# Twelve small ScalarE operations in place of two GpSimd operations, for three of the 24 units of a recurrent-attention and mixture kernel

## The chip, the cores and the metric

The kernel runs on one core of one Trainium2 chip. The metric is the device time of one execution in microseconds (us), the median of several runs. The text calls the engines TensorE (PE in the profile), VectorE (DVE), ScalarE (ACT), GpSimd (POOL) and SyncE (SP, which only issues DMAs here).

## The reference

Three stages follow each other; the inputs are fp32.

```python
batch, n_heads, seq, head_dim = (4, 8, 768, 48)
for t in range(S):
    cur = np.einsum('bhd,bhe->bhde', u[None] * kt, vt)
    y[:, :, t] = np.einsum('bhd,bhde->bhe', rt, state + cur)
    state = wt[:, :, :, None] * state + np.einsum('bhd,bhe->bhde', kt, vt)
# y as x of 3072 x 384
h = x @ w_in                              # 384 x 2048
x = (h * np.clip(h + 3.0, 0.0, 6.0) / 6.0) @ w_out
# soft mixture: 3072 tokens, 32 slots, 8 experts (384 -> 1024 -> 384)
logits = x @ phi
slot_input = softmax(logits over tokens).T @ x
slot_out[e] = np.maximum(slot_input[e] @ w1[e], 0.0) @ w2[e]
out = softmax(logits over slots) @ slot_out
```

Two terms of the first stage matter for the change. The part of `y` from `cur` is a diagonal term: for each token and head, the sum over `d` of `r*u*k`, times `v`. And the state is multiplied by the product of `w` over a chunk of tokens before the next chunk adds to it.

## The kernel before, in words

**Units.** The sequence is cut into six chunks of 128 tokens. A unit `n` is one chunk of one batch: `n = 4*chunk + batch`, 24 units (`UNITS`), counted from 0. `B` is 4 and `SPLIT` is 8. Units 0 to 3 (the first chunk) and most of unit 4 run ahead of the main loop. Units 5, 6 and 7 are the sixth to eighth.

**Steps.** The main loop runs over `s` = 0 to 100. The first 96 are steps of the first matrix product (`mlp(s)`: nine matmuls of 128x512 into `hid`). Every engine has its own copy of the loop and its own fixed order of work. Step `s` belongs to unit and phase `divmod(s + 19, 4)`, so four steps go by for a unit: step 0 is phase 3 of unit 4, steps 1 to 4 are phases 0 to 3 of unit 5, steps 5 to 8 of unit 6, steps 9 to 12 of unit 7, and from step 13 on come the units from 8. All engines run their queues in order, and semaphores with fixed counts tie them together.

**A unit's work.** VectorE scans the decays in both directions (`scan_suffix`, `scan_prefix`; from unit 8 on `open_prefix` with the scan at L962 and `close_suffix` with the scan at L975). GpSimd multiplies keys and receptance by the scans (`decay_keys` L1678, `decay_receptance` L1690). TensorE makes scores (`score`), VectorE masks them (`mask_scores` L1016), ScalarE rounds them to 16 bits (`high_scores` L1380) and GpSimd takes the rest (`low_scores` L1669). `v` is split likewise: `high_v` on ScalarE, `low_v` on VectorE (L1059) for units 4 to 7 and on GpSimd later. `attend` (matmuls from L575) needs the low scores, the low `v` and the decayed state. VectorE adds the diagonal term in `finish_y` (L1035), TensorE turns the result (`turn_x`, L599) and ScalarE and VectorE write it as input of `mlp`. In `increment` TensorE forms what VectorE adds to the state.

**The diagonal term.** GpSimd multiplies `r*k*u` in `diag_products` (L1634, L1636), VectorE sums each head (`sum_diag` L1055, into `diag`, 8 columns), and GpSimd multiplies `v` by it in `diag_values` (L1663, one operation of 128x384, into `diag_v`). `finish_y(n)` waits for it, and SyncE waits for `diag_v_done` before it loads a later unit's natural rows. For units 0 to 3 ScalarE does it with eight operations of 128x48 in `first_diag_values` (L1468), each of which takes one column of `diag` as its scale.

**The state.** For units 4 to 7 GpSimd decays it in `decay_state` (L1705, one operation of 112x384). From unit 8 on ScalarE does, with four operations of 112x96 (`decay_new_state`, L1409).

**The split of the weights.** In the first steps `w_in` is still being split into high and low halves in pieces: ScalarE makes the high one (`high_w`, L1445) and scales the piece (`scale_w`, L1451), behind its work of steps 0, 4, 5, 8 and 9; GpSimd makes the low one (`low_w`, L1648), at the end of its work of steps 1, 2, 5, 6, 9 and 10.

**Per step.** After `mlp(s)`, ScalarE takes `relu_step(s)` (L1473), VectorE `gate(s)` (L1075) and a transpose (L1096); `mlp(s)` needs `gate(s - 2)`. VectorE takes `gate(s)` behind its unit work of the same step.

Of the kernel before, what the change touches and what calls it, by code (L numbers as in the profile page):

```python
# [6 lines left out]
ACT = mybir.ActivationFunctionType  # L7
# [4 lines left out]
P = 128  # L12
# [13 lines left out]
B, H, S, D = 4, 8, 768, 48  # L26
# [3 lines left out]
PB = H // 2  # L30
# [3 lines left out]
PD = ALIGN + D  # L34
# [13 lines left out]
SPLIT = 2 * B  # L48


def build_program(nc, wT, rkT, nat_in_dram, u, u_blocks, w_in, w_outT, w_out, phi, w1, w2, out):
    with ExitStack() as ctx:
        def sb(name, cols, dt=F32):
            return ctx.enter_context(nc.sbuf_tensor(name, [P, cols], dt))

        def sem(name):
            return ctx.enter_context(nc.semaphore(name))
# [4 lines left out]
        def carve(n):  # L62
            at[0] += n
            assert at[0] <= 15872
            return att[:, at[0] - n:at[0]]

        def pairs(ap, n):
            return ap.rearrange("p (i n) -> p i n", n=n)
# [4 lines left out]
        suffix, prefix, restart, mark = (carve(SCAN) for _ in range(4))  # L73
# [11 lines left out]
        diag_v = carve(DM)  # L85
        y_nat = carve(DM)
        state = [pairs(carve(PB * 2 * D), 2 * D) for _ in range(B)]
# [20 lines left out]
        diag = sb("diag", H)  # L108
# [22 lines left out]
        def r_dec_of(n):  # L131
            return r_dec[n % 2 if n < SPLIT else 0]
# [7 lines left out]
        def nat_rows_of(n):  # L140
            return nat_early.get(n, nat[n % 2])
# [25 lines left out]
        def nat_of(n, which):  # L167
            return nat_rows_of(n)[:, which * DM:(which + 1) * DM]
# [89 lines left out]
        state_copied = sem("state_copied")  # L258
        suffix_done = sem("suffix_done")
# [4 lines left out]
        decayed = sem("decayed")  # L264
# [3 lines left out]
        v_scaled = sem("v_scaled")  # L268
# [11 lines left out]
        y_done = sem("y_done")  # L280
# [9 lines left out]
        diag_done = sem("diag_done")  # L290
        diag_v_done = sem("diag_v_done")
# [75 lines left out]
        def unit_of(s):  # L367
            return divmod(s + 4 * B + 3, 4)

        def is_unit(n):  # L370
            return 0 <= n < UNITS

        def scaled_behind(s):
            return {0: 3, 4: 4, 5: 5, 8: 6, 9: 7}.get(s)

        def split_behind(s):
            return {1: 2, 2: 3, 5: 4, 6: 5, 9: 6, 10: 7}.get(s)
# [987 lines left out]
        def _(act):  # L1365
# [23 lines left out]
            def copy_keys(n):  # L1389
                act.wait_ge(k_turned, n + 1)  # L1390
                if n:
                    act.wait_ge(inc_ready, 2 * n)
                scale = Y_SCALE * R_SCALE if n < B else Y_SCALE if n < SPLIT else Y_SCALE / V_SCALE
                nc.scalar.activation(k_nat, k_ps[:, 0:PB * PD], ACT.Copy, scale=scale).then_inc(k_nat_done, 1)
# [9 lines left out]
            def decay_new_state(n):  # L1404
# [4 lines left out]
                    last = nc.scalar.activation(s, s, ACT.Copy, scale=chunk_decay[n % B][0:PD, p:p + 1])  # L1409
                last.then_inc(decayed, 1)  # L1410

            def high_receptance(n):
                act.wait_ge(r_dec_done, n + 1)
                act.wait_ge(y_ready, n)
                nc.scalar.activation(r_hi[0:PD], r_dec_of(n)[0:PD], ACT.Copy).then_inc(r_hi_done, 1)

            def high_state(n):
                if n < SPLIT:
                    act.wait_ge(state_added, n - B + 1)
                else:  # L1420
                    act.wait_ge(decayed, n - B + 1)
                    act.wait_ge(y_ready, n + 1)
                nc.scalar.activation(state_hi[n % B][0:PD], state[n % B][0:PD], ACT.Copy).then_inc(state_hi_done, 1)
# [57 lines left out]
            def copy_logit_parts(g):  # L1481
                act.wait_ge(l_ready, 16 * g + 16)
                if g:
                    act.wait_ge(folded, g)
                if g < C - 1:
                    nc.scalar.activation(l_hi, l_ps[:], ACT.Copy).then_inc(l_hi_done, 1)
                else:
                    nc.scalar.activation(l_part[:, EARLIER], last_l[0], ACT.Copy).then_inc(l_part_done, 1)
                    act.wait_ge(late_l_ready, 4)
                    nc.scalar.activation(l_part[:, LATER], last_l[1], ACT.Copy).then_inc(late_l_part_done, 1)  # L1490
# [57 lines left out]
            for s in range(END):  # L1548
                n, phase = unit_of(s)
                g, i = divmod(s, FT)  # L1550
                if phase == 0:
                    if g >= 1 and i == 1:
                        copy_logit_parts(g - 1)
                    if is_unit(n):
                        high_v(n)
                        if n >= SPLIT:
                            high_receptance(n)
                if phase == 1:
                    if is_unit(n - 1):
                        high_x(n - 1)  # L1560
                    if 1 <= g < C and i == 2:
                        weigh(g - 1)
                    if is_unit(n):
                        high_scores(n)
                if phase == 2:
                    if n < LAST_INC:
                        copy_keys(n)
                    if SPLIT <= n + 1 < UNITS:
                        save_decay(n + 1)
                    if SPLIT - B <= n - 2 < LAST_INC:  # L1570
                        high_state(n - 2)
                if phase == 3 and SPLIT <= n - 1 < LAST_INC:
                    decay_new_state(n - 1)
                if s < STEPS - 1:
                    relu_step(s)
                elif s == STEPS - 1:
                    for half in range(2):
                        last_relu(half)
                if s == 0:
                    copy_keys(B)  # L1580
                c = scaled_behind(s)
                if c is not None:
                    high_w(c)
                    scale_w(c)
                if g == C and i == 2:
                    weigh(C - 1)
                    copy_logits(C - 1)
                if s == STEPS - 10:
                    c_exp(0)
                if s == STEPS - 5:  # L1590
                    c_high(0)
# [7 lines left out]
            for q in range(KT):  # L1599
                cols = slice(q * P, (q + 1) * P)  # L1600
# [14 lines left out]
            for half in range(2):  # L1615
                act.wait_ge(stack_ready, half + 1)
                nc.scalar.activation(stack[0:3 * SLOTS, MODEL[half]], bank[4 + half][0:3 * SLOTS, 0:DM // 2], ACT.Copy,
                                     scale=SLOT_SCALE).then_inc(stack_hi_done, 1)
            for i in range(1, UNITS, 2):
                act.wait_ge(final_ready, i + 1)  # L1620
                if i // 2 >= OUT_PAIRS:
                    act.wait_ge(stored[i // 2 % OUT_PAIRS], 32 if i // 2 % OUT_PAIRS < SINGLE else 16)
                nc.scalar.activation(out_pair[:, i // 2 % OUT_PAIRS, 1, :], bank[4 + i % 4][:, 0:DM], ACT.Copy,
                                     scale=1.0 / (SLOT_SCALE * SOFT_SCALE)).then_inc(final_done[1], 1)

        @block.gpsimd
        def _(pool):
# [73 lines left out]
            def decay_state(n):  # L1701
                pool.wait_ge(suffix_done, n + 1)
                pool.wait_ge(state_copied, n - B + 1)
                s = state[n % B][0:PD]
                nc.gpsimd.tensor_tensor(s, s, pairs(suffix[0:PD, 1:SCAN], P + 1)[:, :, 0:1]  # L1705
                                        .broadcast_to([PD, PB, 2 * D]), ALU.mult).then_inc(decayed, 1)
# [5 lines left out]
            for t in range(2):  # L1712
                last = nc.gpsimd.memset(mask[:, t * P:(t + 1) * P], SCORE_SCALE)
            last.then_inc(ident_step, 1)
            pool.wait_ge(ident_step, 3)
            for t in range(2):
                last = nc.gpsimd.affine_select(out=mask[:, t * P:(t + 1) * P], in_=mask[:, t * P:(t + 1) * P],
                                               compare_op=ALU.is_gt, fill=0.0, base=0, pattern=[[1, P]],
                                               channel_multiplier=-1)
# [18 lines left out]
            for s in range(END):  # L1738
                n, phase = unit_of(s)
                if phase == 0 and is_unit(n):  # L1740
                    diag_products(n)
                    if n >= SPLIT:
                        low_receptance(n)
                if phase == 1:
                    if is_unit(n):
                        low_scores(n)
                if phase == 2:
                    if SPLIT <= n < UNITS:
                        low_v(n)
                    if n + 1 < SPLIT:  # L1750
                        decay_keys(n + 1)
                    elif n + 1 < UNITS:
                        decay_receptance(n + 1)
                if phase == 3:
                    if B < n and n + 1 < SPLIT:
                        decay_receptance(n + 1)
                    elif B < n and n + 1 < UNITS:
                        decay_keys(n + 1)
                    if is_unit(n) and n > B:
                        diag_values(n)  # L1760
                    if n + 1 < SPLIT:
                        decay_state(n + 1)
                    if SPLIT - B <= n - 2 < LAST_INC:
                        low_state(n - 2)
                c = split_behind(s)
                if c is not None:
                    low_w(c)

            cols, tiles = c_parts[0]
# [14 lines left out]
            for q in range(3):  # L1784
                for g in range(EG):
                    first = q * SLOTS + g * 4 * SPE
# [54 lines left out]
```

## Time and profile before

| | |
|---|---|
| median of 3 runs | 411.77 us (411.71 to 412.57) |
| the profiled execution, its own time | 412.07 us |
| its span, first to last instruction | 410.1 us |
| busy TensorE / VectorE / ScalarE / GpSimd | 391.4 / 333.9 / 198.4 / 217.5 us |
| granted TensorE clock, mean | 0.992 |

The profile is of one execution. A busy share is an average over stages with different limits. Matmuls are pipelined: one of 128x512 is shown as 0.38 us although the next starts 0.22 us later, so TensorE can be shown busy in nearly all of a stretch. A row's duration holds the time in which an instruction was held up once it had begun; time before it began is shown as idle.

### The profile page before, as it was taken

The numbers are of one execution on the slowest core, as the hardware profiler recorded it, in microseconds if no ns is written. First come the engines' busy times: TensorE is split into PE (matmuls) and PEld (weight loads), VectorE is DVE, ScalarE is ACT, GpSimd is POOL, SyncE is SP. The second block draws the span as 40 slices with busy tenths as digits, with TensorE's granted clock in tenths as the row PEclk, the third lists the DMA queues.
The fourth block names the chain that finished last, engine by engine and source line by source line (L and its number), as shares of the span: only waits on it lengthen the run. The fifth ranks groups of instructions, "written<-read, shape, count | busy, mean of one in ns | idle before, by whom it ended". The sixth has DMA issues, their size and how long they took to land.

```text
span 410.1 us, 10077 instructions
## 1 busy us (share of the span) xinstructions
PE 391.4 (95%) x3977; PEld 210.0 (51%) x3977; DVE 333.9 (81%) x536; ACT 198.4 (48%) x408; POOL 217.5 (53%) x206
## 2 busy tenths in 40 slices
PE   7999999999999999999999999999999999999981
PEld 3885555455455554555554555554444444543430
DVE  7998799998999898998989998989876887661251
ACT  3576355545545757366554556653533234321141
POOL 2444988978468777658774687775650012010000
PEclk9999999999999999999999999999999999999996
DMA  8999412439242134124430331232007199779929
GB/s 236 336 410 315 135 32 97 125 125 363 74 126 76 53 125 128 39 90 126 127 101 28 126 96 58 100 127 59 2 2 305 21 399 408 238 281 417 391 109 356
DMA packets 16542, 69.36 MB, mean 169 GB/s; under 512 B 2160, under 2 KB 3184, under 8 KB 14832
## 3 DMA queue, kind: packets, MB, share of 16 engines
q1 hardware_dynamic: 16496, 68.73, 48.1%
q8 instruction: 31, 0.51, 0.5%
q14 instruction: 15, 0.12, 0.1%
HBM read 64.00 MB, written 4.72 MB: 168 GB/s over the span
## 4 chain that ended last, share of the span: by engine, by line
PE 57%; issue 14%; POOL 12%; DVE 7%; DMA 5%; ACT 2%; SPq 0%; POOLq 0%; DVEq 0%
PE hid L616 10%; PE hid L617 9%; PE hid L618 9%; DMA att<-rkT_dram 4%; PE l_ps L664 4%; PE l_ps L727 3%; PE sc_ps L500 3%; PE hid L886 3%; POOL w_split L1648 2%; POOL att L1690 2%; DVE att L962 2%; POOL att L1634 1%; PE y_ps L599 1%; POOL att L1678 1%; PE inc_ps L529 1%
## 5 line engine op out<-in xcount | busy, mean ns | idle before, releaser
L1473 ACT ACTIVATE relu<-hid,three 128x512 f32<-128x512 f32 x95 | 65.0, 684 | 93.1 <-PE hid L618 92.8
L616 PE MATMUL hid<-x_split,w_split 128*128 128x512 f16 x285 | 108.3, 380 | 0.7 <-DVE gated L1075 0.7
L618 PE MATMUL hid<-x_split,w_split 128*128 128x512 f16 x285 | 108.0, 379 | 0.0
L617 PE MATMUL hid<-x_split,w_split 128*128 128x512 f16 x285 | 108.0, 379 | 0.0
L1075 DVE SCALAR_TENSOR_TENSOR gated<-relu,hid 128x512 f32<-128x512 f32 x95 | 64.7, 681 | 21.4 <-ACT relu L1473 20.5
L1096 DVE STREAM_TRANSPOSE ring<-gated 128x512 f32<-128x512 f32 x96 | 68.3, 711 | 3.3
L1669 POOL TENSOR_TENSOR att<-att 128x1024 f16<-128x1024 f32 x20 | 41.9, 2096 | 30.0 <-ACT att L1380 30.0
L1678 POOL TENSOR_TENSOR att<-att 112x512 f32<-112x512 f32 x21 | 25.5, 1213 | 43.5 <-DVE att L975 33.9
L616 PEld LDWEIGHTS hid<-x_split,w_split 128*128 128x128 f16 x285 | 27.7, 97 | 37.2 <-DVE gated L1075 6.6
L618 PEld LDWEIGHTS hid<-x_split,w_split 128*128 128x128 f16 x285 | 27.8, 98 | 33.7
L617 PEld LDWEIGHTS hid<-x_split,w_split 128*128 128x128 f16 x285 | 27.9, 98 | 24.6
L1429 ACT ACTIVATE x_split<-y_ps 128x384 f16<-128x384 f32 x24 | 11.8, 490 | 40.5 <-PE y_ps L599 40.5
L500 PEld LDWEIGHTS sc_ps<-att 48*128 48x128 f32 x384 | 23.3, 187 | 9.6 <-issue 8.5
L500 PE MATMUL sc_ps<-att 48*128 48x128 f32 x384 | 27.9, 284 | 0.2 <-POOL att L1678 0.2
L727 PE MATMUL sc_ps<-ring,soft 32*32 32x512 f32 x384 | 26.1, 598 | 0.0
L1380 ACT ACTIVATE att<-att 128x1024 f16<-128x1024 f32 x20 | 21.1, 1057 | 9.8 <-DVE att L1016 8.7
L727 PE MATMUL k_ps<-ring,soft 32*32 32x512 f32 x192 | 25.6, 598 | 0.0
L1690 POOL TENSOR_TENSOR att<-att 112x512 f32<-112x512 f32 x19 | 23.5, 1237 | 3.0 <-DVE att L996 3.0
L1016 DVE TENSOR_TENSOR att<-sc_ps,mask 128x1024 f32<-128x1024 f32 x19 | 22.7, 1195 | 0.5 <-issue 0.5
L962 DVE TENSOR_TENSOR_SCAN att<-att 112x517 f32<-112x517 f32 x16 | 22.7, 1419 | 0.0
L1636 POOL TENSOR_TENSOR att<-att 128x384 f32<-128x384 f32 x20 | 20.9, 1045 | 1.6
L664 PE MATMUL l_ps<-gated,w_phi 128*32 128x512 f32 x160 | 21.3, 605 | 0.0
(299 smaller groups left out, 859.2 us busy)
## 6 DMA issues: line engine op xcount, KB each, us to landing
att<-nat_dram SPq DMA_DIRECT2D x20, 576.0 KB, 4.2
att<-rkT_dram SPq DMA_DIRECT2D x22, 448.0 KB, 5.6
att<-wT_dram SPq DMA_DIRECT2D x22, 226.2 KB, 4.7
att<-w_dram SPq DMA_DIRECT2D x3, 1536.0 KB, 9.9
out_dram<-w_split SPq DMA_DIRECT2D x11, 384.0 KB, 3.9
att<-w_dram SPq DMA_DIRECT2D x5, 768.0 KB, 10.4
stage<-w_in_dram SPq DMA_DIRECT2D x2, 1536.0 KB, 14.0
ring<-w_outT_dram SPq DMA_DIRECT2D x1, 3072.0 KB, 15.5
```

The source lines that it names most:

```text
L500: last = pe.matmul(sc_bank[j][:, cols], k_dec[n % 2][rows, cols], r_dec_of(n)[rows, cols], start=True, stop=True)
L616: pe.matmul(hid[s % 2][:], high, x_high, start=(q == 0), stop=False)
L617: pe.matmul(hid[s % 2][:], high, x_low, start=False, stop=False)
L618: last = pe.matmul(hid[s % 2][:], low, x_high, start=False, stop=(q == KT - 1))
L664: pe.matmul(l_ps[SLOTS * c:SLOTS * (c + 1), :], w_phi[:, i * SLOTS:(i + 1) * SLOTS], gated_tile(g * FT + i), start=(m == 0), stop=(m == 3) ...
L727: ins = pe.matmul(dg_bank_of(g, a)[SLOTS * c:SLOTS * (c + 1), :], weight_T[SLOTS * a:SLOTS * (a + 1), b * SLOTS:(b + 1) * SLOTS], ring_gro ...
L962: nc.vector.tensor_tensor_scan(prefix[0:PD, :], w_rows_of(n)[0:PD, :], mark[0:PD, :], 1.0, ALU.mult, ALU.add).then_inc(prefix_done, 1)
L1075: nc.vector.scalar_tensor_tensor(gated_tile(s), relu_tile(s), 6.0 * GATE, hid[s % 2][:], ALU.min, ALU.mult).then_inc(gated_done, 1)
L1096: nc.vector.transpose(ring_tile(s), gated_tile(s)).then_inc(gated_turned, 1)
L1473: nc.scalar.activation(relu_tile(s), hid[s % 2][:], ACT.Relu, bias=three[:], scale=GATE / H_SCALE)\
L1669: nc.gpsimd.tensor_tensor(scores_lo, scores, scores_hi, ALU.subtract).then_inc(scores_lo_done, 1)
L1690: nc.gpsimd.tensor_tensor(dst, receptance, decay, ALU.mult).then_inc(r_dec_done, 1)
```

## The change

For units 5, 6 and 7 both GpSimd operations move to ScalarE: `diag_values` becomes eight operations of 128x48, behind the `relu_step` of phase 3 (steps 4, 8 and 12), and `decay_state` becomes four operations of 112x96, ahead of the `relu_step` of phase 3 of the unit before (steps 0, 4 and 8). Unit 4's two operations stay on GpSimd. The order of everything else is as it was. The diff is whole:

```diff
@@ scalar, functions @@
+            def decay_old_state(n):
+                act.wait_ge(suffix_done, n + 1)
+                act.wait_ge(state_copied, n - B + 1)
+                for p in range(PB):
+                    s = state[n % B][0:PD, p, :]
+                    first = 1 + p * (P + 1)
+                    last = nc.scalar.activation(s, s, ACT.Copy, scale=suffix[0:PD, first:first + 1])
+                last.then_inc(decayed, 1)
+
+            def loop_diag_values(n):
+                act.wait_ge(diag_done, n + 1)
+                act.wait_ge(y_done, n)
+                if n >= SPLIT:
+                    act.wait_ge(v_scaled, n - SPLIT + 1)
+                for h in range(H):
+                    cols = slice(h * D, (h + 1) * D)
+                    last = nc.scalar.activation(diag_v[:, cols], nat_of(n, 2)[:, cols], ACT.Copy, scale=diag[:, h:h + 1])
+                last.then_inc(diag_v_done, 1)
@@ scalar, loop @@
+                if phase == 3 and n + 1 < SPLIT:
+                    decay_old_state(n + 1)
                 if phase == 3 and SPLIT <= n - 1 < LAST_INC:
                     decay_new_state(n - 1)
                 if s < STEPS - 1:
...
                 if s == 0:
                     copy_keys(B)
+                if phase == 3 and B < n < SPLIT:
+                    loop_diag_values(n)
                 c = scaled_behind(s)
@@ gpsimd, loop @@
-                    if is_unit(n) and n > B:
+                    if is_unit(n) and n >= SPLIT:
                         diag_values(n)
-                    if n + 1 < SPLIT:
-                        decay_state(n + 1)
```

## Rows read from the trace of the kernel before

**Rows 1.** The page: TensorE's busy time, share and instructions.

```profile
PE 391.4 (95%) x3977; PEld 210.0 (51%) x3977; DVE 333.9 (81%) x536; ACT 198.4 (48%) x408; POOL 217.5 (53%) x206
```

**Rows 2.** Busy time of each engine by stretch; first number is its length.

```profile
58.60:72.40 13.80, 13.30 (x116) 7.46 (x115) 13.19 (x18) 8.60 (x13) 11.95 (x10) 1.00 0.32 94
72.40:87.10 14.70, 13.40 (x118) 7.51 (x117) 13.65 (x18) 8.27 (x14) 13.12 (x11) 1.00 0.31 88
87.10:97.70 10.60, 10.60 (x114) 6.19 (x114) 9.91 (x15) 5.13 (x9) 8.50 (x9) 1.00 0.86 340
```

**Rows 3.** Waits of TensorE's matmuls from 42.6 to 110 us: total, times, longest.

```profile
PE y_ps L575 <- DVE att L1059: 1.5, 2, 1.0
PE y_ps L575 <- POOL att L1669: 0.6, 1, 0.6
PE l_ps L727 <- DVE logits L1119: 0.5, 1, 0.5
PE hid L616 <- DVE gated L1075: 0.3, 1, 0.3
```

**Rows 4.** The chain that ended last, around unit 7's attend.

```profile
83.32 0.43 PE y_ps L575 x2
```

**Rows 5.** Timeline of GpSimd: start, duration, then the operation.

```profile
40.15 2.32 POOL L1669 TENSOR_TENSOR att<-att 128x1024 f16<-128x1024 f32 x1
...
70.93 1.18 POOL L1690 TENSOR_TENSOR att<-att 112x512 f32<-112x512 f32 x1 [1.50 <-DVE att L996]
72.07 0.83 POOL L1663 TENSOR_TENSOR att<-att,diag 128x384 f32<-128x384 f32 x1
72.85 0.83 POOL L1705 TENSOR_TENSOR att<-att 112x384 f32<-112x384 f32 x1
73.64 0.86 POOL L1698 TENSOR_TENSOR spare<-att,spare 112x384 f16<-112x384 f32 x1
...
76.52 1.65 POOL L1648 TENSOR_TENSOR w_split<-stage,w_split 128x768 f16<-128x768 f32 x1
78.11 2.93 POOL L1669 TENSOR_TENSOR att<-att 128x1024 f16<-128x1024 f32 x1
81.01 1.64 POOL L1648 TENSOR_TENSOR w_split<-stage,w_split 128x768 f16<-128x768 f32 x1
```

**Rows 6.** Timeline of VectorE.

```profile
39.90 0.71 DVE L1059 SCALAR_TENSOR_TENSOR att<-att 128x384 f16<-128x384 f32 x1
...
72.98 0.56 DVE L1035 SCALAR_TENSOR_TENSOR att<-y_ps,att 128x384 f32<-128x384 f32 x1 [0.81 <-POOL att L1663]
...
76.52 2.74 DVE L962 TENSOR_TENSOR_SCAN att<-att 112x517 f32<-112x517 f32 x1
...
81.62 1.44 DVE L1059 SCALAR_TENSOR_TENSOR att<-att 128x384 f16<-128x384 f32 x1
...
84.33 1.19 DVE L975 TENSOR_TENSOR_SCAN att<-att 112x517 f32<-112x517 f32 x1
```

**Rows 7.** Timeline of ScalarE (xN: N instructions in one row).

```profile
11.86 1.91 ACT L1468 ACTIVATE att<-att,diag 128x48 f32<-128x48 f32 x8
...
38.48 0.67 ACT L1473 ACTIVATE relu<-hid,three 128x512 f32<-128x512 f32 x1
...
55.12 0.69 ACT L1473 ACTIVATE relu<-hid,three 128x512 f32<-128x512 f32 x1 [1.96 <-PE hid L618]
55.70 0.83 ACT L1445 ACTIVATE w_split<-stage 128x768 f16<-128x768 f32 x1
56.57 0.84 ACT L1451 ACTIVATE stage<-stage 128x768 f32<-128x768 f32 x1
...
58.71 0.69 ACT L1473 ACTIVATE relu<-hid,three 128x512 f32<-128x512 f32 x1 [0.88 <-PE hid L618]
...
108.03 1.17 ACT L1409 ACTIVATE att<-att,stats 112x96 f32<-112x96 f32 x4
```

**Rows 8.** ScalarE's line L1468 alone: duration in ns, min/median/max.

```profile
L1468 ACT ACTIVATE att<-att,diag x16: 318/320/335, 11.9 to 20.0; 128x48 f32<-128x48 f32 x16
```

**Rows 9.** SyncE's own waits over the whole run.

```profile
SPq L400 <- POOL att L1663: 221.8, 18, 15.1
```

## The prediction

> **What bounds the kernel now.** I read the page first, then the waits of TensorE, then the stretches around the changed units, and last the timelines of the three other engines there. On the page TensorE is busy 95% of the span and no other engine is above 81% [rows 1]. So a change to other engines pays only where TensorE stands still for them. From 42.6 to 110 us it stands still four times over, 2.9 us in all [rows 3]. The reader should see which of these waits the moved work can reach. The two on `low_v` (L1059) and the one on a gate are 1.8 us, and the stretches place them: TensorE misses 0.50 us of the first and 1.30 us of the second, and nothing of the third [rows 2]. The matmul rows run into each other, by 0.38 against a pitch of about 0.22 us, so each gap is some 0.16 us longer than the rows show. The gap that matters most lies ahead of `attend(7)`, which starts at 83.32 [rows 4].
>
> Why is `low_v(7)` late there? VectorE is itself nearly full, 13.65 of 14.70 us, and GpSimd 13.12 [rows 2]. Two kinds of lost time on VectorE come from GpSimd. One is plain: `finish_y(6)` waits 0.81 us for `diag_values(6)` [rows 6]. The other is inside the durations. The scan takes 1.19 us alone (at 84.33) and 2.74 us at 76.52, where GpSimd begins `low_w(6)` in the same moment; `low_scores(7)`, begun at 78.11 while the scan is at its end, takes 2.93 [rows 5, 6]. Likewise `low_v` takes 0.71 us at 39.90 and 1.44 at 81.62, with `low_w(7)` running since 81.01 [rows 5, 6]. The numbers fit taking turns: scan end 79.26 is `low_w(6)`'s end at 78.17 plus about one scan. So a VectorE operation with both inputs in SBUF and a GpSimd operation do not run together here; whichever began first goes on.
>
> The Trainium skill states this (SBUF — State Buffer, "Who interferes with whom"): a VectorE instruction with two SBUF inputs contends with a GpSimd one that reads SBUF, ScalarE waits for nobody, and the order of issue decides who is blocked. These rows agree, 2.74 against 1.19 us.
>
> That makes a chain of turns in steps 9 to 12: GpSimd's `decay_receptance(7)` at 70.93, then `diag_values(6)`, `decay_state(7)`, `low_state`, `diag_products(7)`, `low_w(6)` to 78.17, the scan to 79.26, `low_scores(7)` to 81.04, `low_w(7)` to 82.65, `low_v(7)` to 83.06 and `attend(7)` at 83.32 [rows 4 to 6]. Two of the links are what the change takes away.
>
> **Removed from GpSimd.** Six operations: three of each kind. By starts, `diag_values` costs 72.85 - 72.07 = 0.78 us and `decay_state` 73.64 - 72.85 = 0.79 us [rows 5], 1.57 us per unit, 4.7 us in all. Only what lies on the chain pays. In the chain above, both do: 1.57 us, if nothing else holds `attend(7)`. The first pair to go (step 0's decay, step 4's diagonal) mostly turns into idle GpSimd time.
>
> **Added on ScalarE: the diagonal values.** Eight operations of this shape take 1.91 us together, 0.24 us each, in a back-to-back row [rows 7]. One alone is shown as 0.32 us [rows 8], so if they did not overlap it would be 2.56 us. I take 1.91, because the row is the same operation with the same operands, and keep 2.56 as the upper bound; a lower one than 1.91 has no ground. They sit behind `relu_step(4)`, `(8)` and `(12)`, as soon as these end, and their inputs (`sum_diag`, `finish_y` of the unit before) are some us old by then.
>
> [...]
>
> **Added on ScalarE: the decays.** Four operations of the nearest form take 1.17 us [rows 7]; there the factor is a column of `stats`, here of `suffix`. Below that I allow 1.1 us (the last one's tail overlaps), above it 4 x 0.36 = 1.45 us. In step 4 they run in the 1.96 us that ScalarE idles ahead of `relu_step(4)` at 55.12 [rows 7], and step 8 is alike: cost nothing. If that cover were gone they would cost 1.17 us each on every gate behind. Step 0 has no cover: `relu_step(0)` at 38.48 [rows 7] directly follows `high_scores(4)`, so it, `gate(0)` and `low_v(4)` at 39.90 [rows 6] come about 1.1 us later. `low_v(4)` then falls into `low_scores(4)`, which runs from 40.15 [rows 5]. It ends near 42.6 instead of 40.6, as much as `low_scores(4)` itself ended before, so `attend(4)`, which already waited 0.6 us for that [rows 3], moves by 0 to 0.2 us. VectorE's further lateness there, 1 to 2 us, meets its idle time before `gate(2)`, whose relu stands behind the turned `x` of unit 4. I take 0.1 us, hidden again by TensorE's 0.5 us gap in the next stretch but one.
>
> **Behind the eight operations.** On ScalarE they are followed in step 4 by `high_w`, `scale_w` (55.70 and 56.57, 1.7 us together), `high_v(6)` and `relu_step(5)`, which stood at 58.71 after 0.88 us idle [rows 7]. Added 1.91, less 0.88: `relu_step(5)` 1.0 us later, at 59.7. It is `gate(5)` that waits for it; VectorE had work before, so the gate moves by some 0.35 us. Against that `finish_y(5)` and `finish_y(6)` no longer wait for GpSimd (0.8 us at the second), and the scan of unit 7 comes when `low_w(4)` is over. Net, I put `low_v(6)` and `attend(6)` 0.2 us earlier, with 0.35 later (at 2.56 us for eight) and 0.5 earlier (the whole gap) as bounds. TensorE itself needs `gate(5)` only four us later.
>
> SyncE's loads wait for the diagonal values [rows 9]. Unit 5's values now end near 55.70 + 1.91 = 57.6 us [rows 7], and unit 6's should end an estimated 2 us before GpSimd's at 72.90 [rows 5], so the loads go out earlier; no gain, since no matmul waits for them in this part [rows 3].
>
> **The sum.** By the chain of turns `attend(7)` starts at 83.32 - 1.57 = 81.75, or 0.3 us sooner if the chain's head does. By TensorE's own work it can't start before 83.32 - 1.30 (the gap of the stretch) - 0.2 (what moved before) = 81.8. Both say 1.5 us. From 87.1 on TensorE is full [rows 2] and all that follows hangs on its progress, so 1.5 us reach the end. The later wait of 0.5 us [rows 3] starts from TensorE's own work and stays. For the profiled execution: 412.07 - 1.5 = 410.6 us. It was 0.3 us above the median, so for the median 411.77 - 1.5 = 410.3 us.
>
> **The rivals.**
>
> *More is given back.* If all gaps that the waits show in this part close (1.8 us, and 0.16 us each in the three), and part of the later 0.5 us because VectorE runs ahead, it is 2.4 us: 409.4 us. For it: VectorE's wait at `finish_y` and its lost turns both go. Against it: after `low_w(7)` there is always `low_v(7)`.
>
> *VectorE instead of GpSimd.* The queue on ScalarE delays `relu_step(5)` and `(9)`; VectorE stays in order, so scans, masks and `low_scores` follow it, and GpSimd's free time is just idle. Worked with 1 us of gate delay kept at unit 7 instead of 0.3 gained, `attend(7)` gains 0.3 to 0.7 us: 411.3 us. For it: VectorE is 13.19 of 13.80 us busy [rows 2]. Against it: it was 0.8 us idle for exactly this result.
>
> *Slower: lost turns at step 0.* `low_v(4)` behind `low_scores(4)`, then `low_w(1)` on VectorE behind `diag_values(4)`, then the scan of unit 6 behind `low_w(2)` (up to 1.6 us). VectorE would reach step 2 some 2.5 us late, `attend(5)` slip by as much, less what its `low_v` has to spare, and the 1.5 us won later would not cover it: +0.9, 412.7 us. It decides from the point at which `gate(2)` is over 1.5 us late. For it: the step has no cover on ScalarE, and one `low_w` or scan is a whole turn. Against it: GpSimd runs 0.8 us ahead there, so `low_w(2)` should be over.
>
> **How the numbers follow.** Forecast 0.52, more 0.14, VectorE's pace 0.22, slower 0.12. The forecast's own range is 409.8 to 410.9. The whole range is 409.3 to 412.0: down to the second case, up over the third; it leaves out the slower one and little else. A measurement of this kernel can tell about 0.2%, 0.8 us, from no change. Faster by more takes the first two cases and a little of the third: 0.68. Within it: 0.20. Slower: 0.12.
>
> **What would show it.** Right: GpSimd's two lines are gone between 45 and 88 us, the scan at L962 for unit 8 is near 1.3 us, `finish_y(6)` has no wait on GpSimd, TensorE misses under 0.4 us instead of 1.3 in the stretch that ends with `score(8)`, and `attend(7)` starts near 81.8. Wrong: eight operations over 2.2 us, a new wait of VectorE on `relu_step(5)` or `(9)` over 1 us, `gate(2)` later than 52.5, or another scan near 2.7 us.

## The result and the profile after

The changed kernel takes 410.12 us (median of 19 runs) against 411.72 us before (19 runs beside them). The ratio is 0.9965, with a 95% interval of 0.9953 to 0.9977: 1.4 us faster, at least 0.9 and at most 1.9. In a later set of runs (10 against 27) the ratio was 0.9949 (0.9927 to 0.9971). The profiled execution took 409.8 us, its span 408.1 us against 410.1.

The page, with each engine's busy time: GpSimd has lost six instructions and 7.3 us, ScalarE has gained 36 and 8.0 us. The six operations were 4.7 us by their starts. The other 2.6 us of GpSimd, and the 2.2 us by which VectorE's busy time fell with the same 536 instructions, went out of rows that stayed: they are shorter now.

```profile
PE 391.7 (96%) x3977; PEld 210.6 (52%) x3977; DVE 331.7 (81%) x536; ACT 206.4 (51%) x444; POOL 210.2 (52%) x200
```

The stretches of [rows 2] in the changed kernel, in the same columns:

```profile
58.60:72.40 13.80, 13.73 (x124) 7.89 (x125) 12.87 (x20) 11.95 (x27) 10.20 (x8) 1.00 0.37 103
72.40:87.10 14.70, 14.70 (x137) 8.14 (x133) 13.29 (x21) 10.57 (x24) 12.19 (x11) 1.00 0.38 121
87.10:97.70 10.60, 10.60 (x103) 5.74 (x100) 9.20 (x14) 5.31 (x10) 7.89 (x8) 1.00 0.95 361
```

TensorE is now busy in all of the stretch in which it missed 1.30 us. Its waits from 42.6 to 110 us, against [rows 3], with the two on `low_v` and the one on the gate gone:

```profile
PE y_ps L575 <- DVE att L1059: 0.8, 1, 0.8
PE l_ps L727 <- DVE logits L1119: 0.5, 1, 0.5
```

The one of 0.8 us is another one: it is `attend(4)`, which waited for GpSimd before. GpSimd's timeline of the same work as in [rows 5] (the change added lines ahead of GpSimd's functions, so their line numbers are higher by 23):

```profile
39.91 1.99 POOL L1692 TENSOR_TENSOR att<-att 128x1024 f16<-128x1024 f32 x1
...
70.47 1.18 POOL L1713 TENSOR_TENSOR att<-att 112x512 f32<-112x512 f32 x1 [1.50 <-DVE att L996]
71.61 0.86 POOL L1721 TENSOR_TENSOR spare<-att,spare 112x384 f16<-112x384 f32 x1
...
74.47 1.66 POOL L1671 TENSOR_TENSOR w_split<-stage,w_split 128x768 f16<-128x768 f32 x1
76.98 2.02 POOL L1692 TENSOR_TENSOR att<-att 128x1024 f16<-128x1024 f32 x1 [0.86 <-ACT att L1380]
78.97 1.64 POOL L1671 TENSOR_TENSOR w_split<-stage,w_split 128x768 f16<-128x768 f32 x1
```

And VectorE's, against [rows 6]:

```profile
40.58 1.74 DVE L1059 SCALAR_TENSOR_TENSOR att<-att 128x384 f16<-128x384 f32 x1
...
71.63 0.52 DVE L1035 SCALAR_TENSOR_TENSOR att<-y_ps,att 128x384 f32<-128x384 f32 x1
...
75.87 1.34 DVE L962 TENSOR_TENSOR_SCAN att<-att 112x517 f32<-112x517 f32 x1
...
79.77 1.25 DVE L1059 SCALAR_TENSOR_TENSOR att<-att 128x384 f16<-128x384 f32 x1
```

`finish_y(6)` has no idle time ahead of it, and the scan for unit 8 takes 1.34 us where it took 2.74: `low_w(6)` ends at 76.13, and the scan began only 0.26 us before that. `low_scores(7)`, 2.93 us before, takes 2.02 and now has idle time ahead. `low_v(7)` is still held by `low_w(7)`, but both come about 2 us earlier, and `attend(7)`, with no wait ahead of it, starts at 81.33 in place of 83.32 [rows 4].

ScalarE, against [rows 7]: the four decays ahead of `relu_step(0)`, and in step 4 the eight operations with what follows them.

```profile
38.21 1.16 ACT L1418 ACTIVATE att<-att 112x96 f32<-112x96 f32 x4
39.27 0.67 ACT L1492 ACTIVATE relu<-hid,three 128x512 f32<-128x512 f32 x1
...
53.02 1.16 ACT L1418 ACTIVATE att<-att 112x96 f32<-112x96 f32 x4
55.08 0.69 ACT L1492 ACTIVATE relu<-hid,three 128x512 f32<-128x512 f32 x1 [0.90 <-PE hid L618]
55.66 1.90 ACT L1428 ACTIVATE att<-att,diag 128x48 f32<-128x48 f32 x8
...
59.49 0.67 ACT L1492 ACTIVATE relu<-hid,three 128x512 f32<-128x512 f32 x1
```

VectorE's waits from 34 to 110 us show the price of that queue. Two gates waited for ScalarE before, 2.2 us in all, and now 8 do, 4.7 us. Against that `finish_y` waited 2.4 us for GpSimd before and has no such wait now. The two rows before, then the one after:

```profile
DVE att L1035 <- POOL att L1663: 2.4, 4, 0.8
DVE gated L1075 <- ACT relu L1473: 2.2, 2, 1.7
```

```profile
DVE gated L1075 <- ACT relu L1492: 4.7, 8, 1.1
```

**A measure for the experiments.** A single execution's time differs from the next by 1 us and more, and a part of that is already there before the changed work begins. So each profile is also read by one stretch: from the start of the suffix scan of unit 5 (the first operation at L984 after 33 us) to the start of `score(8)` (L500). Before it is 87.08 - 34.85 = 52.23 us, after 85.03 - 34.59 = 50.44 us: 1.79 us shorter. From `score(8)` to the span's end it is 323.0 us before and 323.1 after. So all of the gain arises in this stretch, and the other 0.26 us by which the spans differ were there at its start. In the experiments below this last part is 323.0 or 323.1 us too, but for *the change in all units*, where it is 324.0. The stretch is read from one profile for each row of the table; the kernel before was profiled once, the changed kernel twice (50.44 and 50.46).

### The profile page after: what moved, and what is told of

It reads as the page before. It is cut to its first block, busy times and chain, and to the rows that moved or that the text cites. A ratio compares the mean times of both kernels' runs of the same rounds, so it can differ in the third digit from the quotient of the medians.

```text
span 408.1 us, 10107 instructions
## 1 busy us (share of the span) xinstructions
PE 391.7 (96%) x3977; PEld 210.6 (52%) x3977; DVE 331.7 (81%) x536; ACT 206.4 (51%) x444; POOL 210.2 (52%) x200
## 4 chain that ended last, share of the span: by engine, by line
PE 70%; issue 10%; DVE 8%; POOL 6%; ACT 3%; DMA 1%; POOLq 0%; DVEq 0%; ACTq 0%
PE hid L616 11%; PE hid L617 11%; PE hid L618 11%; PE l_ps L664 4%; PE sc_ps L500 4%; PE l_ps L727 3%; PE hid L886 3%; PE y_ps L599 2%; PE inc_ps L529 2%; PE hid L651 2%; PE k_ps L510 1%; PE hid L867 1%; PE sc_ps L867 1%; PE sc_ps L727 1%; PE y_ps L575 1%
## 5 line engine op out<-in xcount | busy, mean ns | idle before, releaser
L1692 POOL TENSOR_TENSOR att<-att 128x1024 f16<-128x1024 f32 x20 | 40.0, 2001 | 35.0 <-ACT att L1380 35.0
L500 PEld LDWEIGHTS sc_ps<-att 48*128 48x128 f32 x384 | 23.3, 187 | 9.5 <-issue 8.3
L500 PE MATMUL sc_ps<-att 48*128 48x128 f32 x384 | 27.9, 284 | 0.2 <-POOL att L1701 0.2
L727 PE MATMUL sc_ps<-ring,soft 32*32 32x512 f32 x384 | 26.1, 598 | 0.0
L727 PE MATMUL k_ps<-ring,soft 32*32 32x512 f32 x192 | 25.6, 598 | 0.0
L588 PE MATMUL y_ps<-att 128*128 128x48 f16 x160 | 21.0, 185 | 0.0
```

The source lines that it names most:

```text
L500: last = pe.matmul(sc_bank[j][:, cols], k_dec[n % 2][rows, cols], r_dec_of(n)[rows, cols], start=True, stop=True)
L727: ins = pe.matmul(dg_bank_of(g, a)[SLOTS * c:SLOTS * (c + 1), :], weight_T[SLOTS * a:SLOTS * (a + 1), b * SLOTS:(b + 1) * SLOTS], ring_gro ...
L1692: nc.gpsimd.tensor_tensor(scores_lo, scores, scores_hi, ALU.subtract).then_inc(scores_lo_done, 1)
```

## Experiments

| kernel | stretch, us | to before | median, us (before beside it) | ratio, 95% interval |
|---|---|---|---|---|
| before | 52.23 | | | |
| the change | 50.44 | -1.79 | 410.12 (411.72) | 0.9965 (0.9953 to 0.9977) |
| diagonal values alone | 51.04 | -1.19 | 410.80 (411.83) | 0.9984 (0.9964 to 1.0005) |
| decays alone | 51.04 | -1.19 | 411.01 (411.83) | 0.9987 (0.9975 to 1.0000) |
| the change, GpSimd's load kept | 51.60 | -0.63 | 411.27 (411.83) | 0.9988 (0.9973 to 1.0003) |
| the change, decay of unit 5 later | 50.21 | -2.02 | 409.92 (411.83) | 0.9949 (0.9936 to 0.9961) |
| the change, eight operations twice | 53.49 | +1.26 | 413.13 (411.91) | 1.0034 (1.0018 to 1.0050) |
| the change in all units | 50.46 | -1.77 | 411.13 (411.91) | 0.9977 (0.9961 to 0.9993) |
| the change again | 50.46 | -1.77 | 409.44 (411.56) | 0.9949 (0.9927 to 0.9971) |
| decay of unit 5 later, again | 50.92 | -1.31 | 409.39 (411.56) | 0.9945 (0.9925 to 0.9965) |
| low scores of unit 4 first | 50.33 | -1.90 | 410.04 (411.56) | 0.9971 (0.9945 to 0.9996) |

The medians go the way of the stretch, but the intervals of most of these kernels overlap, and those of the diagonal values alone and of the kept load reach past 1. So the times alone don't tell the two halves, or the kept load, apart: what follows rests on the stretch and on rows.

**Which half brings it?** Only the diagonal values on ScalarE:

```diff
-                if phase == 3 and n + 1 < SPLIT:
-                    decay_old_state(n + 1)
...
+                    if n + 1 < SPLIT:
+                        decay_state(n + 1)        # GpSimd
```

> Only the diagonal values move to ScalarE; the three decays stay on GpSimd. Measure: from the start of the suffix scan of unit 5 (34.85 us before, 34.59 after) to the start of score(8) (87.08, 85.03), 52.23 us before and 50.44 with the whole change. Theory of turns (the gain is GpSimd work taken out of the chain that VectorE's scan and low_v take turns with): about half of GpSimd's 1.57 us per unit is gone, no cost at step 0, so the stretch is 51.1 to 51.4 us and the time 0.8 to 1.1 us below before. Rival (the gain is VectorE's wait for the diagonal values, 0.8 us a unit, with the decays irrelevant): the stretch is 50.2 to 50.5 us and the time at least 1.7 us below before.

And only the decays on ScalarE:

```diff
-                if phase == 3 and B < n < SPLIT:
-                    loop_diag_values(n)
...
+                    if is_unit(n) and n > B:
+                        diag_values(n)            # GpSimd
```

> Only the three decays move to ScalarE; the diagonal values stay on GpSimd. Theory of turns: 0.79 us less GpSimd work per unit in the chain, less 0.2 us lost at step 0: stretch 51.5 to 51.8 us (52.23 before), time 0.4 to 0.7 us below before. Rival (VectorE's wait for the diagonal values is what counts): the wait stays, step 0 costs 0.2, so stretch 52.2 to 52.4 us and no gain.

Both shorten the stretch by 1.19 us. The first is near what the theory of turns said (51.04 against 51.1 to 51.4), the second gained more than it said (51.5 to 51.8). Neither rival came: the first wanted 50.2 to 50.5, the second 52.2 to 52.4. With the decays alone `finish_y` still waits for GpSimd as before:

```profile
59.26 0.56 DVE L1035 SCALAR_TENSOR_TENSOR att<-y_ps,att 128x384 f32<-128x384 f32 x1 [0.22 <-POOL att L1684]
...
72.51 0.56 DVE L1035 SCALAR_TENSOR_TENSOR att<-y_ps,att 128x384 f32<-128x384 f32 x1 [0.81 <-POOL att L1684]
...
76.04 1.96 DVE L962 TENSOR_TENSOR_SCAN att<-att 112x517 f32<-112x517 f32 x1
```

So the wait that [rows 6] show ahead of `finish_y(6)` can stay and most of the gain still comes. It is GpSimd's 0.79 us less that lets `low_w(6)` begin at 75.25 and the scan lose 0.8 us in place of 1.55. The halves don't add up to the whole, since with both TensorE is full: in either half `attend(7)` keeps a wait of 0.6 us, with both it has none.

**Load or wait?** The whole change, and GpSimd does two multiplications of the same shapes into unused columns of `acc`, where the two operations stood; nothing uses what they write.

```diff
+            def idle_multiply(rows, first):
+                nc.gpsimd.tensor_tensor(acc[0:rows, first:first + DM], u_all[0:rows], u_all[0:rows], ALU.mult)
...
+                    if B < n < SPLIT:
+                        idle_multiply(P, 3 * DM)
+                    if n + 1 < SPLIT:
+                        idle_multiply(PD, 4 * DM)
```

> The whole change, but GpSimd does two multiplications of the same shapes into unused columns where the two moved operations stood, so its queue is as long as before while nothing waits for these two. They add work whose results nothing uses. Theory of turns: the scan of unit 8 still takes over 2.5 us and attend(7) waits for low_v(7) as before; stretch 52.0 to 52.4 us, time within 0.4 us of before. Rival (the waits for the results count, the load does not): stretch 50.4 to 50.7 us, time as with the whole change.

Neither number came: 51.60 us, 0.63 less than before and 1.16 more than the change. GpSimd's load is therefore the larger part, and the waits for its results are a part too. The rows show how the smaller part arises. GpSimd's second multiplication of `diag_products(7)` and `low_w(6)` in this kernel, and then the scan:

```profile
75.70 1.00 POOL L1659 TENSOR_TENSOR att<-att 128x384 f32<-128x384 f32 x1
76.66 2.58 POOL L1671 TENSOR_TENSOR w_split<-stage,w_split 128x768 f16<-128x768 f32 x1
```

```profile
76.05 1.75 DVE L962 TENSOR_TENSOR_SCAN att<-att 112x517 f32<-112x517 f32 x1
```

Without the wait at `finish_y(6)` VectorE reaches the scan 0.4 us earlier, and now it is ahead of `low_w(6)`. The same pair meets as in the kernel before, but in the other order: there the scan took 2.74 us and `low_w(6)` 1.65, here 1.75 and 2.58. What the scan still loses here goes to the multiplication that was running when it began: it ends 1.09 us after that one's end at 76.70. My sharp version of the theory, that only the load counts, falls: who comes first is part of it. The end of GpSimd's queue then sets the time. `score(8)` waits 0.69 us for the decayed keys.

**Step 0.** The decay of unit 5's state moves behind `relu_step(1)`:

```diff
-                if phase == 3 and n + 1 < SPLIT:
+                if phase == 3 and B < n and n + 1 < SPLIT:
                     decay_old_state(n + 1)
...
+                if s == 1:
+                    decay_old_state(B + 1)
```

> The whole change, but the decay of unit 5's state stands behind relu_step(1) instead of ahead of relu_step(0), where ScalarE has 6 us of idle time. Theory (ahead of relu_step(0) it pushes gate(0) and low_v(4) into low_scores(4), and attend(4) 0.2 us back): stretch 50.2 us (50.44 with the whole change), gate(0) has no wait, time 0.2 us below the whole change. Rival (attend(4) waits for low_scores(4) on GpSimd anyway, nothing lost): stretch 50.4 us, same time as the whole change.

The stretch is 50.21 us, as expected, `gate(0)` has no wait, and `attend(4)` starts 7.75 us after the scan in place of 7.99 (7.77 in the kernel before). Whether the time follows could not be told from two sets of runs made apart, so both kernels ran once more beside each other.

> The changed kernel once more, beside the next two on the same chip: 1.4 to 1.8 us below the kernel before, stretch from unit 5's suffix scan to score(8) 50.4 us.

> The kernel with the decay of unit 5 behind relu_step(1) once more: stretch 50.2 us, 0.2 us below the changed kernel, if the loss at step 0 is real; the same as the changed kernel if it is not.

Side by side the medians are 409.44 and 409.39 us: 0.2 us is below what the runs resolve, and the expected 0.2 us less is neither confirmed nor excluded. The changed kernel is 2.1 us below the kernel before in this set (1.2 to 3.0 by the interval), where 1.4 to 1.8 was expected; its stretch is 50.46, as expected. The stretch of the second profile of the later decay, 50.92 us, missed its 50.2, and the edit is not the reason. In this execution unit 5's input came late, the decays (`wT`) first:

```profile
35.91 1.23 DVE L984 TENSOR_TENSOR_SCAN att<-att 112x517 f32<-112x517 f32 x1 [1.17 <-DMA att<-wT_dram]
...
42.22 1.99 POOL L1694 TENSOR_TENSOR att<-att 128x1024 f16<-128x1024 f32 x1
```

The scan began 1.17 us late and GpSimd followed. A late scan alone would not lengthen a stretch that starts at the scan. But the next load, of the keys and the receptance (`rkT`), issued at 17.91, took 19.8 us to land, against 17.3 in the first profile, and `decay_keys(5)`, which waits for it, began 0.70 us after the scan's end in place of 0.08. So `low_scores(4)`, at 42.22, ended 8.30 us after the scan's start in place of 7.61, which is the 0.7 us of the stretch. The profile puts `attend(4)`'s wait of 2.55 us there down to ScalarE's decays, which end at about the same time. But `attend(4)` waits for no decay of unit 5. It starts 0.15 us after the end of `low_scores(4)`, just as in the kernel before (40.15 + 2.32 = 42.47 [rows 5], start 42.62). From `attend(4)` to `score(8)` it is 42.47 us here, 42.46 in the first profile of this kernel and 42.45 with the change; before it was 44.46.

**How much does ScalarE have left?** Each unit's eight operations are done a first time into unused columns.

```diff
+                for dst in (acc[:, 3 * DM:4 * DM], diag_v):
+                    for h in range(H):
```

> The whole change, with each unit's eight operations of the diagonal values done a first time into unused columns, so ScalarE has 1.9 us more ahead of high_w and of relu_step(5), (9) and (13). Theory of ScalarE's slack (it is used up: with the change gate(5) and gate(9) already wait 0.4 and 0.7 us for their relu, and every further us goes to VectorE and by unit 7 to TensorE): relu_step(9) 1.9 us later, attend(7) 1.2 to 1.8 us later than with the change, stretch 51.6 to 52.3 us. Rival (TensorE is the bound with room to spare, gates have two steps of slack): stretch 50.4 to 50.7 us, time as with the change.

It is worse than the theory's figure of 51.6 to 52.3: 53.49 us, 3.05 more than the change, for three times 1.9 us. The gates wait 1.52 us for their relu in steps 5 and 9, `finish_y` waits for ScalarE by 0.3 to 0.6 us, and a wait that I had not priced comes on top, TensorE's `increment` for the keys that ScalarE copies, queued behind the rest:

```profile
PE y_ps L575 <- DVE att L1059: 1.9, 3, 0.8
PE inc_ps L529 <- ACT att L1394: 1.6, 2, 1.2
```

**The same change where TensorE is full.** The diagonal values of units 8 to 23 go to ScalarE too.

```diff
-                if phase == 3 and B < n < SPLIT:
+                if phase == 3 and B < n and is_unit(n):
                     loop_diag_values(n)
```

> The whole change, and the diagonal values of units 8 to 23 on ScalarE too, in the same place. Before, finish_y waited 7.0 us in 11 times for GpSimd's diagonal values, but from 87 us on TensorE is full. Theory (no gain where TensorE is full; a loss where the eight operations stand ahead of the logit parts' copy at each chunk's end, which lies on the chain): time equal to the whole change or up to 1.5 us above it. Rival (VectorE's 0.8 us waits count in the later units as well): 1 us or more below the whole change.

The stretch is as with the change. From `score(8)` on it loses: from `score(9)` to `score(23)` it is 195.48 us against 194.54. That is within what the theory said, and the rival's gain did not come. Of the loss 0.14 to 0.15 us comes at each of the four chunk ends in this part, and 0.35 between `score(20)` and `score(21)`. At the first chunk end the copy of the logit parts (L1505) starts at 97.00 in place of 96.84, right behind the eight operations, and the chain goes on from that copy; what makes the 0.35 is open. The rows of the first:

```profile
95.19 1.90 ACT L1428 ACTIVATE att<-att,diag 128x48 f32<-128x48 f32 x8
97.00 0.57 ACT L1505 ACTIVATE soft<-l_ps 128x512 f16<-128x512 f32 x1
```

**The next wait ahead.** `attend(4)` still waited 0.6 us for GpSimd. On GpSimd `low_scores(4)` was put between the two multiplications of `diag_products(4)`, on top of the later decay.

```diff
                 nc.gpsimd.tensor_tensor(rku, nat_of(n, 0), nat_of(n, 1), ALU.mult).then_inc(rk_done, 1)
+                if n == B:
+                    low_scores(B)
                 pool.wait_ge(rk_done, n - B + 1)
```

> As the last one, and on GpSimd low_scores(4) stands between the two multiplications of diag_products(4), not behind both, since attend(4) still waits 0.6 us for it. Theory (what comes ahead of attend(4) is still GpSimd's queue, and TensorE is full from there to score(8)): low_scores(4) ends 1 us earlier, attend(4) starts 0.4 to 0.6 us earlier, stretch 49.6 to 49.8 us, and 0.4 to 0.6 us less in all. Rival (VectorE, whose sum_diag(4) and low_v(4) now come later, is late next and takes it back by attend(5)): stretch 50.1 to 50.4 us, no gain.

The rival was right: 50.33 us. `score(5)` starts 9.93 us after the scan of unit 5 in place of 10.56, so 0.6 us are won at first. But VectorE's `low_w(1)` now falls among three GpSimd operations, and by `score(6)` the lead is gone (23.89 us after the scan, 23.74 without the edit). `attend(5)` waits 0.2 us for `low_v(5)`, which it didn't before. VectorE's row, then GpSimd's in the same time:

```profile
42.85 3.19 DVE L1065 SCALAR_TENSOR_TENSOR w_split<-stage,w_split 128x768 f16<-128x768 f32 x1
```

```profile
42.31 1.18 POOL L1717 TENSOR_TENSOR att<-att 112x512 f32<-112x512 f32 x1
43.45 0.83 POOL L1690 TENSOR_TENSOR att<-att,diag 128x384 f32<-128x384 f32 x1
44.23 1.00 POOL L1659 TENSOR_TENSOR att<-att 128x384 f32<-128x384 f32 x1
```

## Why the prediction was right, point by point

- **What bounds the kernel.** Right. The gain is TensorE's idle time ahead of `score(8)`, and from there the rest of the span is as long as before (323.0 and 323.1 us). The loads of units' natural rows go out earlier, as said (57.63 in place of 59.10 us and 70.70 in place of 72.96), and no matmul here waited for them either time.
- **The turns.** Right in kind. The scan for unit 8 was to take about 1.3 us and takes 1.34, `finish_y(6)` does not wait, and keeping GpSimd's load gives back 1.16 of 1.79 us. Too narrow was the claim that the two moved operations pay by their durations, 1.57 us: either alone, 0.8 us, brings 1.19. With both, `low_v(7)` ends at 81.02 in place of 83.06 us, 2.04 sooner, and 0.3 us ahead of `attend(7)`. Of the two bounds that the sum made equal, the chain's and TensorE's, it was TensorE's that held.
- **ScalarE's prices.** Right. Eight operations 1.90 us (1.91), four decays 1.16 us (1.17), and `relu_step(5)` at 59.49 where 59.7 was said. The bound of 2.56 us for eight, which takes the operations one by one, is not what a row of eight costs here. They start every 0.225 us; the 0.24 of the prediction is the row's length by eight and counts the last one's tail. The Trainium skill (ScalarE: Activation LUTs, "What ACT_TABLE_LOAD costs") gives 280 ns + 0.833 ns per column for an operation with one operand of a value per partition, 0.32 us at 48 columns, and says that such operations back to back overlap by about 93 ns. An estimate from these figures is 8 x 0.32 - 7 x 0.093 = 1.91 us, and the trace agrees with 1.90.
- **Step 0.** Right in kind, larger in size: `low_v(4)` fell into `low_scores(4)` (1.74 us in place of 0.71) and `attend(4)` came 0.22 us later in the stretch's measure, where I took 0.1 within 0 to 0.2. Placed one step later the decay costs nothing there. VectorE's lateness was used up ahead of `gate(2)`, as said: it waits 1.13 us there in place of 1.75.
- **`attend(6)`.** 0.2 us earlier was said. `score(7)` starts 0.21 us earlier in the measure, but as -0.43 (of the gap of 0.50 that the rows show, 0.07 is left at `attend(6)`) and +0.22 from step 0. That they sum to the 0.2 said is in part luck, since step 0 had been put at 0.1.
- **The sum.** 1.5 us said; 1.79 in the profile's stretch, 1.4 by the ratio and 2.1 in the later set. Both intervals hold 1.5 and 1.79, so that 1.4 lies so near the forecast says little. The term that was too small is what TensorE could recover ahead of `attend(7)`. I took the 1.30 us that its busy rows leave open. From `score(7)` to `score(8)` it is 14.67 us before and 13.09 after, 1.58 us. The rest, 0.28 us, is what the rows hide. From start to start TensorE regains 1.16 us ahead of `attend(7)`, shown as a wait of 1.01, and 0.36 behind `increment`, shown as 0.29; from `attend(7)` to `score(8)` it is 0.06 us shorter. I had named 0.16 us for each gap and left it out of this bound.
- **The rivals.** *More is given back* (2.4 us) did not come: the gaps closed, but the 0.5 us at L727 stays, as the sum assumed, and step 0 takes 0.2. *VectorE instead of GpSimd* did not come, though it is near: gates wait 4.7 us for ScalarE (2.2 before), and 1.9 us more per unit on ScalarE turn the gain into a loss of 1.26 us. *Slower by lost turns at step 0* did not come; `low_w(2)` was over (48.58 us) when the scan had lost only 0.6 us.

## What to carry to other kernels

Where two engines hold each other up, look for it inside the durations, not among the waits: a row that takes 2.7 us here and 1.2 there names the other engine by what began before it. Work taken from the one then pays on the other, even if nobody waits for its result, up to the point where the engine that sets the pace is full; count that room from start to start, since a pipelined engine's rows hide part of each gap. The engine that takes the work over needs idle time at that very place in its order: put it one step later where there is some, and stop where the pace-setter has no gap left.

## What the runs showed of the hardware

- A VectorE operation with two inputs in SBUF and a GpSimd one take turns, and either can lose: `low_w(6)` took 1.65 us where it was ahead of the scan and 2.58 where the scan was ahead. In nine of the eleven profiles GpSimd was in an operation when the scan for unit 8 began (in the kernel before, `low_w(6)`, begun in the same moment). There the scan's length goes from 1.34 to 2.74 us, but it always ends 1.09 or 1.10 us after that operation. In the other two, the eight operations twice and the low scores first, GpSimd was in none, and the scan took 1.23 us.
- I had expected one turn to be lost at most. `low_w(1)` on VectorE took 3.19 us in the last experiment, against 0.94 in the changed kernel, where it began ahead of GpSimd's next operation. So it lost 2.25 us, as much as more than two of the operations that GpSimd ran meanwhile: it ended 0.81 us after the third of the rows shown. The Trainium skill says that whichever starts first gets the shared port pair for the whole instruction and the other fully blocks (SBUF — State Buffer, "SBUF: two separate sides"). The two orders of the scan and `low_w(6)` agree with it. Why `low_w(1)`, already waiting, lost again to the next two of GpSimd's, where the waiting scan of the kept load went ahead of the next, stays open.
- Eight ScalarE operations of 128x48 with a column as scale start every 0.225 us, though each is shown as 0.32; four of 112x96 every 0.27 us, each shown as 0.36.
- Executions of one kernel differ by 1 us and more, as much as this change brings. One source was seen once: the loads for unit 5 came late, the decays 1.17 us after VectorE was ready for them. What makes the rest was not found.
